# Three small constant tiles of a fused retention and MLP kernel are allocated ahead of the shared staging region instead of behind it

## The reference

```python
# q, k, v: (4, 8, 768, 64); gamma[h] = 1 - 2**(-5-h)
for t in range(S):
    state = gamma * state + einsum('bhd,bhe->bhde', k[:, :, t], v[:, :, t])
    y[:, :, t] = scale * einsum('bhd,bhde->bhe', q[:, :, t], state)
x = y.transpose(0, 2, 1, 3).reshape(3072, 512)
h = x @ w_in;  x = (h * cos(h)) @ w_out            # 512 -> 2048 -> 512
h = x @ w_in2; g = where(h >= 1, h, where(h <= -1, 0, (h + 1)**2 / 4))
return g @ w_out2
```

## Time and profile before

| | us |
|---|---|
| device time, median of 3 runs | 1135.67 |
| lowest and highest | 1134.82, 1136.92 |
| the profiled execution, own time | 1134.82 |
| its span, first to last instruction | 1133.0 |
| PE busy in the span | 1089.4 (96%) |
| DVE, ACT, POOL busy | 706.6, 506.2, 261.4 |
| mean granted TensorE clock | 0.991 |

### The profile page before, as it was taken

How to read it: one execution, slowest core, us unless ns; L and a number is a source line. 1 busy time by engine, 2 the same in 40 slices (tenths; PEclk the granted TensorE clock), 3 DMA queues, 4 the chain that set the end, 5 groups by cost and what they waited for, 6 DMA issues and landing times.

```text
span 1133.0 us, 14409 instructions
## 1 busy us (share of the span) xinstructions
PE 1089.4 (96%) x5572; PEld 891.3 (79%) x5572; DVE 706.6 (62%) x1016; ACT 506.2 (45%) x822; POOL 261.4 (23%) x251
## 2 busy tenths in 40 slices
PE   7789999999999999999998899999999999999998
PEld 5668777777888788788876788887888887888887
DVE  4677675464766546466658677756566647566632
ACT  2367775234666523466654454434333344333232
POOL 6366652320000121000028665504000004000000
PEclk8989999999999999999999999999999999999999
DMA  9235554433333343333223634443233331233111
GB/s 348 101 110 197 204 186 149 149 100 152 130 116 108 133 137 94 139 131 129 85 94 112 234 120 158 167 167 139 102 130 131 111 121 74 103 130 130 66 38 38
DMA packets 44452, 149.12 MB, mean 132 GB/s; under 512 B 4704, under 2 KB 4832, under 8 KB 42336
## 3 DMA queue, kind: packets, MB, share of 16 engines
q1 hardware_dynamic: 44384, 148.20, 36.5%
HBM read 106.24 MB, written 41.94 MB: 131 GB/s over the span
## 4 chain that ended last, share of the span: by engine, by line
PE 68%; DVE 13%; ACT 9%; POOL 3%; DMA 3%; issue 3%; SPq 1%; DVEq 0%; ACTq 0%
PE bank L488 10%; PE bank L492 10%; PE bank L490 10%; PE bank L521 7%; PE bank L523 7%; PE bank L522 7%; PE bank L517 5%; DVE g_lo L713 4%; PE bank L518 4%; PE bank L519 4%; ACT work L926 2%; ACT work L928 2%; DVE x_lo L655 2%; DMA kn_sb<-in_k_n 2%; PE bank L401 2%
## 5 line engine op out<-in xcount | busy, mean ns | idle before, releaser
L488 PE MATMUL bank<-x_hi,tw 128*128 128x512 f32 x672 | 264.5, 394 | 12.1 <-ACT work L899 4.3
L492 PE MATMUL bank<-x_hi,tw 128*128 128x512 f32 x672 | 262.8, 391 | 0.0
L490 PE MATMUL bank<-x_lo,tw 128*128 128x512 f32 x672 | 262.8, 391 | 0.0
L517 PE MATMUL bank<-g_hi,wd_hi 128*128 128x512 f32 x384 | 154.1, 401 | 10.6 <-DVE g_lo L713 9.5
L488 PEld LDWEIGHTS bank<-x_hi,tw 128*128 128x128 f32 x672 | 126.8, 189 | 44.0 <-DVE late L704 5.3
L521 PE MATMUL bank<-wd_hi,g_hi 128*128 128x512 f32 x384 | 150.1, 391 | 0.7 <-DVE g_lo L713 0.7
L518 PE MATMUL bank<-g_lo,wd_hi 128*128 128x512 f32 x384 | 150.4, 392 | 0.0
L519 PE MATMUL bank<-g_hi,wd_lo 128*128 128x512 f32 x384 | 150.3, 391 | 0.0
L522 PE MATMUL bank<-wd_lo,g_hi 128*128 128x512 f32 x384 | 149.5, 389 | 0.0
L523 PE MATMUL bank<-wd_hi,g_lo 128*128 128x512 f32 x384 | 149.4, 389 | 0.0
L492 PEld LDWEIGHTS bank<-x_hi,tw 128*128 128x128 f32 x672 | 126.9, 189 | 26.6
(11 more groups left out here) (91 smaller groups left out, 1466.3 us busy)
## 6 DMA issues: line engine op xcount, KB each, us to landing
tw<-t_scratch SPq DMA_DIRECT2D x64, 896.0 KB, 6.4
t_scratch<-tw SPq DMA_DIRECT2D x16, 1792.0 KB, 7.6
work<-x_scratch SPq DMA_DIRECT2D x24, 256.0 KB, 3.6
raw<-in_w1u SPq DMA_DIRECT2D x16, 256.0 KB, 3.1
wd_raw<-in_w1d SPq DMA_DIRECT2D x8, 512.0 KB, 8.6
q_sb<-in_q_t SPq DMA_DIRECT2D x16, 256.0 KB, 3.0
k_sb<-in_k_t SPq DMA_DIRECT2D x16, 256.0 KB, 4.0
v_sb<-in_v_n SPq DMA_DIRECT2D x16, 256.0 KB, 4.2
```

Of the source, the lines that this page charges most:

```text
L488: nc.tensor.matmul(to[:, :], w[:, kt, 0, i, :], x_hi[:, i, kt, :], start=opens, stop=False, skip_group_check=True)
L490: nc.tensor.matmul(to[:, :], w[:, kt, 0, i, :], x_lo[:, i, kt, :], start=False, stop=False, skip_group_check=True)
L492: last = nc.tensor.matmul(to[:, :], w[:, kt, 1, i, :], x_hi[:, i, kt, :], start=False, stop=kt == 1, skip_group_check=True)
L517: nc.tensor.matmul(to[i][:, :], wd_hi[:, f, cols], g_hi[:, slot, :], start=opens, stop=False)
```

## The change

The three allocations are asked for ahead of `shared` instead of behind it.

```diff
         state = sb("state", [P, KT, B, P])
+        tb = sb("tb", [P, TABLE_WIDTH])
+        half_one = sb("half_one", [P, 1])
+        probe = sb("probe", [P, 1])
+
 
 
         quad_size = 2 * 2 * 7 * P * 4
...
         kn_sb = nc.alloc_sbuf_tensor_at("kn_sb", [P, N], F32, offset=place + 8 * N * 4)
-        tb = sb("tb", [P, TABLE_WIDTH])
-        half_one = sb("half_one", [P, 1])
-        probe = sb("probe", [P, 1])
```

## The result

| | before, us | after, us |
|---|---|---|
| median (4 runs each) | 1135.24 | 1145.99 |
| lowest to highest | 1133.66 to 1136.92 | 1143.63 to 1147.88 |
| profiled execution: own time, span | 1134.82, 1133.0 | 1146.63, 1144.8 |

The ratio is 1.0094, with a 95% interval of 1.0067 to 1.0119. No change was forecast (range 1133.5 to 1137.9), so the prediction was wrong. The two profiled spans differ by 11.8 us.

What follows compares the result with a forecast made beforehand. The prediction took TensorE's matmul step of about 227 ns to bound the kernel. Every term was taken as 0, so the profiled span stayed 1133.0 us and the forecast median 1135.6 us, range 1133.5 to 1137.9.

Steps and rivals of the forecast that it cites:

- What bounds the kernel: TensorE, busy 96% of the span and 68% of the chain, sets the pace at about 227 ns a step.
- No instruction, order or wait changes; only the offset modulo 256 is new: Whole kernel: added and removed work sum to nothing; tiles in `shared` move from 128 past a multiple of 256 onto one.
- TensorE reads of `tw`: I take 0: Product matmuls: weight loads from the moved tile keep their 188 to 189 ns, so no change in time.
- a slower load costs nothing until it has grown by 39 ns: Product weight loads: each idles 39 ns beside the preceding matmul, the 227 ns step less the 188 ns load.
- The bounds: Ends for TensorE's product matmuls: 4.0 us gained to 216 us lost, over 2016 of them.
- rival 1: DMA loads into `shared` get quicker by starting on a 256-byte line: 1.1 us gained, 1134.6 us; chance 0.20.
- rival 3: Retention stages: nine `kn_sb` loads land later, up to 10.8 us lost, 1146.5 us; chance 0.07.
- Rival 2: Product matmuls: TensorE's step gets shorter, 2 ns each giving 1131.6 us; chance 0.06.
- Writes and reads by the other engines: 0: DVE, ACT and GpSimd accesses to moved tiles: no change, with ends of 0.1 us over 32 mask writes.
- DMAs: Transfers into and out of `shared`: no change taken, between 1.1 us gained and 10.8 us lost.
- the prediction's ninth: `kn_sb` loads: a 2048-byte row costs eight 256-byte lines instead of nine, saving 0.08 us of 0.75 us a load.
- The chances: Whole kernel: 0.87 for within 0.2%, 0.06 for faster by more, 0.07 for slower by more.

Runs made afterwards that it cites:

- e2: Kernel before the change, with 128 bytes of padding ahead of `shared` and `tb` still behind it: 1147.63 us, ratio 1.0105.
- e1: Kernel after the change, with 128 bytes of padding between `probe` and `shared`, restoring the old remainder of `shared`: 1135.38 us, ratio 0.9994.
- e9: Separate kernel of TensorE matmuls alone, operand start distance varied by stretch: 60 float32 steps took 13.60 us at distance 0, 14.00 at 128.
- e3: Kernel before the change, with 128 bytes of padding ahead of the very first tile, so all start on multiples of 256: 1132.21 us, ratio 0.9971.
- e7: Kernel before the change, with 64 bytes of padding ahead of `shared`: 1148.08 us, ratio 1.0116.
- e8: Kernel before the change, with 32 bytes of padding ahead of `shared`: 1147.14 us, ratio 1.0108.

## Why the prediction was wrong

*What bounds the kernel* was right: TensorE's step sets the pace, and it is what lost the time.

*No instruction, order or wait changes; only the offset modulo 256 is new* was right. e2 shows that 128 bytes on `shared` are enough for the whole loss, and e1 that it goes when they are given back.

*TensorE reads of `tw`: I take 0* is the step that failed. Its reason was that 188 to 189 ns came back for every tile and block. The text itself said that all tiles started at 128 past a multiple of 256; so the sameness over tiles showed nothing on the one bit that moved, nor on the distance between two operands, which was a multiple of 256 in every long matmul of the trace. In its place the runs showed a step of 232.5 ns where weights and moving operand differ in that remainder, 5.8 ns by 2016. The sentence that "a slower load costs nothing until it has grown by 39 ns" looked at the wrong quantity: the weight load grew by about 1 ns in the mean, and the slack behind it from 39 to 43 ns (29.1 us over 672), while the step grew by 5.8. So the load was not what set the step, and its slack shielded nothing; a load that is slower by more was never tried. That the two reads of TensorE disturb each other would fit, but it is argued: no run shows what holds the step up. The Trainium skill, "SBUF — State Buffer", section "Who interferes with whom", says that the weight load and the moving operand have independent read ports and that TensorE waits for no one. In time the two are not independent in e9, with 14.00 against 13.60 us for the same 60 matmuls; whether the ports are the place isn't shown.

*The bounds*: 4.0 us of gain to 216 us of loss held the 11.7, but the range left them out: it was made of the spread of three runs, rival 1 and the foot of rival 3. Rival 2 named the right place and the right leverage, 1.1 ns on 2016 matmuls making 2.3 us, and looked only to the fast side, though its bound was open to both.

*Writes and reads by the other engines: 0* was right (ACT 506.3 us after 506.2, POOL 261.6 after 261.4; the mask writes stay hidden). DVE is busy 3.2 us longer, nearly all of it in the 192 operations that write `g_lo` (870 and 877 ns before, 887 and 892 after), which touch no moved tile. These vary from run to run without a tie to the starts: with the remainders of the kernel after, e2 has 855 and 896 ns.

*DMAs, and rival 1* (a gain of 1.1 us by the 256-byte line): not seen. `kn_sb` lands in 2.6 against 2.7 us in the median, but packets of 2048 bytes, the size of its rows, take 84 ns in the median before and in e3, where every tile starts on a multiple of 256; a ninth of that would be 9 ns. By the rule of the Trainium skill cited in the prediction, reads that start on a line should have cost less. The stores are the reads out of `tw`, and their packets take 535 ns in the median with `tw` at 128, at 0 and at 160 past a multiple. The rule as the page has it is also cheaper than the prediction's ninth: by its count of beats, an estimate, a row of 2048 bytes would save 4 of 68 beats and one of 14336 bytes 4 of 452, 5 ns of 535. The traces have no such 5 ns.

*Rival 3* (slower, by `kn_sb` landing later) had the right sign and the wrong mechanism; the `kn_sb` loads on the chain took 2.55 to 2.80 us, where they had taken 2.55 to 2.74, and the loop kept its 7.04 us within 0.01.

*The chances*: 0.07 for slower rested on one mechanism, rival 3, that the runs don't show. The case for a loss in TensorE was missing.

## What to carry to other kernels

Where float32 matmuls (declared `F32R`) with 512 columns follow one another, start the tiles of weights and of moving operands at the same remainder of 256 bytes (and slice them at multiples of 256): in this kernel a difference of 32 bytes already cost 1%. An allocation added in front of a region can break it without any sign in instructions or waits and with weight loads as short as before, so compare the step from start to start by line. And if every row of a trace has one property in common, the trace says nothing on what happens without it, so the range has to be as wide as the leverage of that step.

## What the runs showed of the hardware that was not expected

- Step of a float32r matmul (128x128 weights, 512 columns) in an unbroken stream, at a granted clock of 1.00, the level of 2.4 GHz: 227 ns with equal remainders of 256 bytes, 233 to 234 ns with the moving operand 32, 96, 128, 160, 192, 224 and 384 bytes higher than the weights, 232 at 16, 229 at 64 (e9). In the kernel, with the moving operand 192 and 224 past the weights modulo 256, it was 233 ns (e7, e8).
- It needs no other engine, DMA or tile (e9). Half of the weights apart costs as much as all, 13.99 against 14.00 us for 60.
- In bfloat16 the distances of 0, 32, 128 and 256 made no difference, 216 ns (e9).
- The median time of a DMA packet did not depend on where its row starts in SBUF, at 0, 32 or 128 past a multiple of 256 among others: 84 ns for 2048 bytes, 272 for 7168, 535 for 14336 (before, after, e2, e3, e8).
- Why the step gets longer is not shown by any run here; only the condition is. Matmuls with fewer columns, and those of the retention, whose tiles are declared `F32`, were not measured for it.
